# Unused bytes between the weight buffers of an attention-and-two-MLPs kernel

## What is computed

```python
qn = q / (norm(q, axis=1) + 1e-06);  kn = k / (norm(k, axis=1) + 1e-06)
s = kn.transpose(0, 2, 1) @ qn / tau              # 256 x 256 for each batch
a = softmax(s, -1)                                # with 1e-9 added to the sum
x = (v @ a).reshape(12160, 256)
x = (np.maximum(x @ moe_w_in, 0) ** 2) @ moe_w_out
x = (np.maximum(x @ moe2_w_in, 0) ** 2) @ moe2_w_out
```

## Time and profile before

| | |
|---|---|
| median of 2 runs | 2197.22 us (2196.42 to 2198.01) |
| the profiled execution | 2196.81 us, its span 2194.7 us |
| TensorE matmul | busy 2179.6 us (99%), 9836 records |
| TensorE weight load | busy 1826.6 us (83%), 9836 records |
| VectorE | busy 1252.9 us (57%) |
| ScalarE | busy 1018.1 us (46%) |
| mean granted TensorE clock | 0.998 of 2.4 GHz |
| DMA | 60.94 MB, mean 28 GB/s |

### The profile page before, as it was taken

The page is one execution under the profiler, slowest core; times in us unless marked ns, Lnnn a source line. Parts: engine busy times, 40 slices in busy tenths (PEclk is TensorE's granted clock), DMA queues, the critical chain, the costliest instruction groups (busy, mean ns, idle before and its releaser), DMA issues.

```text
span 2194.7 us, 29614 instructions
## 1 busy us (share of the span) xinstructions
PE 2179.6 (99%) x9836; PEld 1826.6 (83%) x9836; DVE 1252.9 (57%) x1875; ACT 1018.1 (46%) x1722; POOL 3.2 (0%) x10
## 2 busy tenths in 40 slices
PE   8999999999999999999999999999999999999998
PEld 7888888888888888888888888888888888888887
DVE  6765555555565555656655555555555555555544
ACT  5554444444444454444544444444444444444443
POOL 0000000000000000000000000000000000000000
PEclk9999999999999999999999999999999999999999
DMA  8310001100011000112111010110110101101001
GB/s 294 96 49 20 19 19 25 33 19 19 19 29 29 19 19 20 33 23 49 37 20 19 1 20 0 19 19 0 19 18 1 19 0 19 19 0 18 10 1 19
DMA packets 215874, 60.94 MB, mean 28 GB/s; under 512 B 199281, under 2 KB 203377, under 8 KB 215825
## 3 DMA queue, kind: packets, MB, share of 16 engines
q1 hardware_dynamic: 215824, 60.31, 11.7%
HBM read 47.84 MB, written 12.45 MB: 27 GB/s over the span
## 4 chain that ended last, share of the span: by engine, by line
PE 99%; DVE 0%; DMA 0%; ACT 0%; issue 0%; DVEq 0%; SPq 0%
PE bank L321 32%; PE bank L323 32%; PE bank L322 32%; PE bank L455 2%; PE bank L402 0%; DMA qk<-in_k 0%; PE bank L416 0%; DVE s_acc L818 0%; PE bank L410 0%; DVE stats L822 0%; DVE rawl L713 0%; DVE out_sb L726 0%; ACT s_acc L592 0%; ACT rawh L521 0%; DVEq L90 0%
## 5 line engine op out<-in xcount | busy, mean ns | idle before, releaser
L747 DVE TENSOR_TENSOR g_sb<-r_sb 128x512 f32<-128x512 f32 (+1 forms) x768 | 527.3, 687 | 896.6 <-ACT r_sb L545 890.4
L545 ACT ACTIVATE r_sb<-bank 128x512 f32<-128x512 f32 (+1 forms) x768 | 456.0, 594 | 1109.3 <-PE bank L323 1102.1
L713 DVE TENSOR_TENSOR gl<-g_sb,gh 128x512 fp32r<-128x512 f32 (+1 forms) x768 | 519.7, 680 | 0.5 <-DVE g_sb L747 0.5
L533 ACT ACTIVATE gh<-r_sb 128x512 fp32r<-128x512 f32 (+1 forms) x768 | 470.7, 619 | 0.0
L321 PE MATMUL bank<-yh,w2h 128*128 128x512 f32 (+1 forms) x768 | 297.8, 388 | 0.0
L321 PE MATMUL bank<-xh,w1h 128*128 128x512 f32 (+1 forms) x768 | 297.4, 387 | 0.0
L322 PE MATMUL bank<-yl,w2h 128*128 128x512 f32 (+1 forms) x768 | 297.4, 387 | 0.0
L322 PE MATMUL bank<-xl,w1h 128*128 128x512 f32 (+1 forms) x768 | 297.4, 387 | 0.0
L321 PE MATMUL bank<-gh,o2h 128*128 128x512 f32 (+1 forms) x768 | 297.3, 387 | 0.0
L323 PE MATMUL bank<-yh,w2l 128*128 128x512 f32 (+1 forms) x768 | 297.3, 387 | 0.0
L323 PE MATMUL bank<-gh,o2l 128*128 128x512 f32 (+1 forms) x768 | 297.3, 387 | 0.0
(11 more groups left out here) (101 smaller groups left out, 1623.8 us busy)
## 6 DMA issues: line engine op xcount, KB each, us to landing
v_sb<-in_v SPq DMA_DIRECT2D x88, 128.0 KB, 3.0
out<-out_sb SPq DMA_DIRECT2D x88, 128.0 KB, 2.5
raw<-in_q SPq DMA_DIRECT2D x22, 256.0 KB, 2.7
raw<-in_k SPq DMA_DIRECT2D x22, 256.0 KB, 3.0
qk<-in_q SPq DMA_DIRECT2D x10, 512.0 KB, 5.2
qk<-in_k SPq DMA_DIRECT2D x10, 512.0 KB, 6.3
w_early<-in_moe_w_in SPq DMA_DIRECT2D x4, 512.0 KB, 6.0
xT<-in_moe_w_out SPq DMA_DIRECT2D x4, 512.0 KB, 3.9
```

Of the source, the lines that this page charges most:

```text
L533: nc.scalar.activation(gh[:, f % SLOTS, 0:n], r_sb[:, f % 2, 0:n], ACT.Square).then_inc(gh_done, 1)
L545: nc.scalar.activation(r_sb[:, f % 2, 0:n], h_ps[f % SLOTS][:, 0:n], ACT.Relu)\
L713: return nc.vector.tensor_tensor(dst, x, as32(hi), ALU.subtract)
L747: nc.vector.tensor_tensor(g_sb[:, f % 2, 0:n], r, r, ALU.mult).then_inc(sq_done, 1)
```

## The change

Five unused buffers are allocated between the weight buffers. No instruction is added, removed or moved: on every engine the program holds the same instructions in the same order.

```diff
             w_early = sb("w_early", [P, PIECES, PIECE], scope=early)
+        sb("pad_w2", [P, 48])
         w2h, w2l = sb("w2h", [P, CB, F], f32r), sb("w2l", [P, CB, F], f32r)
+        sb("pad_o2", [P, 88])
         o2h, o2l = sb("o2h", [P, NF, C], f32r), sb("o2l", [P, NF, C], f32r)
+        sb("pad_w1", [P, 8])
         w1h, w1l = sb("w1h", [P, CB, F], f32r), sb("w1l", [P, CB, F], f32r)
+        sb("pad_o1", [P, 48])
         o1h, o1l = sb("o1h", [P, NF, C], f32r), sb("o1l", [P, NF, C], f32r)
+        sb("pad_x", [P, 64])
         xh, xl = sb("xh", [P, CB, TILE], f32r), sb("xl", [P, CB, TILE], f32r)
```

## The result

The changed kernel takes 2237.67 us (median of 2 runs, 2237.21 to 2238.13) against 2197.22 us, a ratio of 1.0184 with a 95% interval of 1.0167 to 1.02. It is slower by 40 us, many times the spread of the runs. The forecast was no change, 2197 us, with a range up to 2225; the time lies 13 us above that range. The profiled span grew from 2194.7 to 2236.4 us.

The account below looks back on a forecast made before the run. The prediction took TensorE's matmul stream, one 512-column start every 226.7 ns, as the bound. Every term was 0 (the fold 1 us at most, either way), so 2196.81 us + 0 = 2197 us, range 2090 to 2225 us.

Parts of the forecast that it names:

- nothing but the distance between matmuls could move the time: Whole stages: TensorE never waits there, so only the start-to-start distance, 226.7 ns for 512 columns, can change the time.
- the instructions: All engines and queues: none added, removed or moved, so 0 us.
- the early part: Before the stages: early buffers stay in place, and what overlays them is still written after them, so 0 us.
- the fold: 96 matmuls with `w1h`, `w1l` as moving data: 1 us at most, either way.
- the other engines: ScalarE and VectorE use moved buffers at other addresses; ScalarE's idle 1109.3 us would cover any cost: 0 us.
- the excess of 10.8 ns: Stage matmuls: float32r starts every 226.7 ns against 215.9 for the float32 logits; the excess shows only at full clock.
- I take 0: The 8448 + 768 stage matmuls: distance unchanged by the new offsets, 0 us, between 103 us less and 83 us and over more.
- Equal rests are the bad case: Rival, stage matmuls: weight and moving reads collide at equal rests; full relief gives 2094 us; chance 0.33 for over 2% faster.
- The settled state is lost: Rival, stage matmuls: offset switches every six unsettle the stream, 2220 to 2240 us; chance 0.15 over 2% slower, 0.12 within.
- some 3590: Sign in the profile after: matmuls in an 830 us stretch if the settled state is lost; 3663 was the forecast.
- bigger losses (under 0.15): Range choice: its upper end, 2225 us, stops where small losses end and leaves these out.
- stay at 120 ns in any case: Sign at batch 1's 256-column logits: distance must hold since their relation is unchanged; if it moves, offset isn't the cause.

Follow-up runs that it names:

- u16: Kernel before, padded so that all four weight pairs start 16 bytes above the moving data, modulo 512: 2197.77 us, ratio 1.0003.
- map3: Kernel before plus streams behind its last stage, at several offsets after 256-column matmuls or a settled stream, and in the kernel's own pattern; no total time given.
- u64: Kernel before, padded so that all four weight pairs start 64 bytes off the moving data, modulo 512: 2252.26 us, ratio 1.0249.
- map1: Kernel before plus streams of 24 float32r matmuls behind its last stage, weight start moved in 16-byte steps, some with other column counts; no total time given.
- map2: Kernel before plus streams behind its last stage: fewer weight columns, 256 moving columns, offsets switching every six matmuls, or plain float32; no total time given.
- u496: Kernel before, padded so that all four weight pairs start 496 bytes (16 below) off the moving data, modulo 512: 2256.61 us, ratio 1.0269.
- u128: Kernel before, padded so that all four weight pairs start 128 bytes off the moving data, modulo 512: 2246.03 us, ratio 1.0223.

## Why the prediction was wrong

**What held.** That nothing but the distance between matmuls could move the time: yes, 3591 in the stretch, waits and other engines as before. That the instructions, the early part, the fold and the other engines give 0: yes, to about 1 us. The folds took 1.4 us more in the profiled execution, 1.2 of it because 14 matmuls of the first fold came at the 427 ns of 1.2 GHz in place of 8; u16, whose time didn't change, had 13 of them. That the excess of 10.8 ns is a matter of float32r data at full clock: the float32 streams, with no offset effect at all, agree.

**The step that failed** is "I take 0" for the matmuls of the stages. Its reason was that in the rows the excess "follows the history of the stream, not where operands lie". The first half is right, and map3 shows how much so. The second half had no support: all rows had one relation, so they couldn't speak about another, as the text itself said a paragraph earlier. The runs showed in its place 3.4 to 6.3 ns more on each of the 8448 matmuls, 40 us, because three of the four new relations have a longer distance of their own and the fourth can't settle beside one of them. History and relation aren't rivals: the relation decides which lasting patterns there are, the history which of them is taken.

**The rivals.** "Equal rests are the bad case" was the wrong way round: with 512 columns offset 0 is among the best of the map, and no offset reached the 216 ns that this rival's 2094 us stood on. "The settled state is lost" came nearest. It named the size, 4.7 ns for each matmul from the earlier trace rows, 2240 us and "some 3590" matmuls in the stretch; measured 2237.67 and 3591. But its 2240 us laid the loss on the switches alone, and u64, without a switch, loses 55 us; longer settled distances it named only as the condition for a loss beyond 2%. Its premise that the matmuls with 448 columns never settle doesn't hold for a stream of its own either: in map1 they settle at 206.7 ns, more than the 202.7 of the stages. By map1 and the start times the loss divides like this: own distances 2112 x (6.4 + 6.7 + 2.2) = 32 us for `w1`, `o2` and `w2`; the other 8 us are switches, above all at `o1`, which stands between `w1` at 64 and costs 3.5 ns more than alone. That the total met a price taken from unsettled distances is in part luck: those, and the patterns at bad offsets, are made of the same single distances between 226 and 238 ns.

**The numbers.** I left a loss beyond 2225 us out of the range as "bigger losses (under 0.15)". But the very rows on which the rival rested gave 30 to 43 us, and the upper end of an unknown cost belongs into the range: with it, 2240, the range would have held. The rows of the batch-1 logits were to "stay at 120 ns in any case"; their mean went from 120.1 to 119.7 ns with the same relation as before. That test was ill made, since the matmuls ahead of them had changed, and with them their history.

**The rule of the Trainium skill** that I weighed, independent read ports for moving data and weights ("TensorE: Matmul & The Clock Gate", "Step-by-step: what each phase is for"), has it that the term is 0. The runs disagree in effect: 233.3 against 226.7 ns for two addresses of the weights. Nor does the excess go with the bytes of a weight load, since 32 columns do no better than 128.

**What stays open.** What inside the chip is shared, and why the settled distance is 226.7 at best and not 216. The runs show the relation (period 256 bytes), its absence at half rate, and the lasting patterns; they don't show the part that makes them. Many of the settled means (200.0, 206.7, 226.7, 233.3, 240.0 ns) are whole multiples of 6.67 ns, the time of 16 columns at 2.4 GHz; why is open as well. No version beat the kernel before: for 128 weight columns and 512 moving columns it already has the best relation of the map. For its 768 matmuls with 448 columns it hasn't (`w2` at 192 has 200.4 to 200.7 ns there in place of 202.7), but they are too few to matter: at 2 ns each, less than 2 us.

## What to carry to other kernels

In a dense stream of float32r matmuls at full clock, the start of the weights relative to the moving data, modulo 256 bytes, was worth up to 3% of the matmul time. With 128 weight columns and 512 moving columns, 0 was as good as any and reached its best state from every past that was tried, so equal rests are the place to start from for this shape. They aren't a rule for others: with 256 moving columns offset 0 was the slowest of four, with 448 columns and with 96 weight columns another offset was faster. Measure before padding. In a profile, look for such a loss in the number of matmuls in a stretch: the waits and the busy shares look the same, and the recorded durations grow by a few ns only. And when every row of a trace has the same value of what a change alters, the trace can't say that it doesn't matter; price it from the nearest disturbed rows, and keep that price in the range.

## What the runs showed of the hardware

- Float32r, 128 x 128 weights, 512 columns at 2.4 GHz: 226.7 ns from start to start at offsets 0 and 256, 233.1 to 233.7 at 32 to 64 and 128 to 160, 228.9 at 192 (map1). Float32 data: 429.2 ns at each of the four offsets tried (map2).
- With 256 moving columns: 120.0 ns at offset 0, 117.8 at 64 and at 192 (map2). Offset 0 with 320 and 384 columns: 146.7 and 173.3 ns; with 128 and 192 columns some 112 ns (map1).
- A stream of 36 matmuls at offset 16 ran at 226.7 ns after a settled stream and at 233.3 after matmuls of 256 columns (map3). The kernel stays at 226.7 in its stages with offset 16 (u16) and at 233.3 with 496 (u496), where a stream at 496 had 226.7 or 228.3.
- The excess doesn't fall with the weight bytes: 96, 64 or 32 columns of weights gave 226.7 to 240.0 ns (map2).
- With 448 columns single distances went down to 195 and up to 212 ns (u128); means of streams ranged from 200.0 to 206.7 (map1).
